# Attention products on two halves of TensorE's columns, in a fused linear-attention and MoE kernel

## What is computed

```
# r, k, v: (4, 8, 768, 48) = batch, head, time, head_dim; w, u: (8, 48)
for t in range(S):
    cur = einsum('bhd,bhe->bhde', u * k_t, v_t)
    y_t = einsum('bhd,bhde->bhe', r_t, state + cur)
    state = w * state + einsum('bhd,bhe->bhde', k_t, v_t)
x = y as 3072 tokens of 384 features
h = max(x @ w1, x @ w2, x @ w3)            # 384 -> 768
x = h @ w_out                              # 768 -> 384
xn = x / sqrt(mean(x * x) + 1e-6) * rms_g
out = (silu(xn @ w_gate) * (xn @ w_val)) @ w_out2     # 384 -> 1536 -> 384
```

## Time and profile before

| | us |
|---|---|
| median of 3 runs | 930.51 |
| lowest and highest run | 929.02, 930.55 |
| span of the profiled execution, first to last instruction | 927.3 |
| TensorE busy in it | 890.9 |
| VectorE, ScalarE, POOL busy | 439.4, 334.9, 156.6 |

### The profile page before, as it was taken

One profiled execution on the slowest core, in us unless ns is written; L12 is line 12 of the kernel. 1 busy time (PEld: TensorE's weight loads), 2 busy tenths in 40 slices (PEclk: granted clock), 3 DMA queues, 4 the chain that ended last, 5 costly groups with the idle time before them and its releaser, 6 DMA issues.

```text
span 927.3 us, 15577 instructions
## 1 busy us (share of the span) xinstructions
PE 890.9 (96%) x5428; PEld 884.9 (95%) x5428; DVE 439.4 (47%) x1053; ACT 334.9 (36%) x790; POOL 156.6 (17%) x197
## 2 busy tenths in 40 slices
PE   3689999999999999999999999999999999999998
PEld 3579999999999999999999999999999999999998
DVE  7976565546555565644532524234342432424321
ACT  2453333434334333333445324333243332433322
POOL 5552223232212223200334100000000000000000
PEclk9779999999999999999999999999999999999999
DMA  7263113122311312103232000000000000000000
GB/s 238 92 213 112 58 56 115 55 62 65 103 54 55 112 54 77 37 6 102 69 80 58 17 10 1 27 1 27 0 0 25 0 25 0 0 25 0 25 1 26
DMA packets 44406, 48.28 MB, mean 52 GB/s; under 512 B 3536, under 2 KB 38224, under 8 KB 44368
## 3 DMA queue, kind: packets, MB, share of 16 engines
q1 hardware_dynamic: 44368, 47.79, 16.5%
HBM read 41.88 MB, written 4.72 MB: 50 GB/s over the span
## 4 chain that ended last, share of the span: by engine, by line
PE 91%; DVE 6%; issue 2%; ACT 0%; DMA 0%; DVEq 0%; ACTq 0%
PE h_b L409 16%; PE h_b L411 16%; PE h_b L410 16%; PE y_b L409 8%; PE y_b L411 8%; PE y_b L410 8%; PE a_b L395 4%; PE s_b L380 4%; PE s_b L409 3%; PE s_b L410 3%; PE s_b L411 3%; PE a_b L399 2%; DVE kd L773 2%; PE a_b L403 1%; DVE xl L807 1%
## 5 line engine op out<-in xcount | busy, mean ns | idle before, releaser
L409 PE MATMUL h_b<-xh,Wh 128*128 128x384 f32 x648 | 225.8, 348 | 4.1 <-DVE xl L807 4.1
L411 PE MATMUL h_b<-xh,Wl 128*128 128x384 f32 x648 | 217.8, 336 | 0.0
L410 PE MATMUL h_b<-xl,Wh 128*128 128x384 f32 x648 | 217.7, 336 | 0.0
L409 PE MATMUL y_b<-hh,Wh 128*128 128x384 f32 x432 | 144.5, 334 | 0.4 <-DVE hl L982 0.3
L411 PE MATMUL y_b<-hh,Wl 128*128 128x384 f32 x432 | 144.6, 335 | 0.0
L410 PE MATMUL y_b<-hl,Wh 128*128 128x384 f32 x432 | 144.3, 334 | 0.0
L409 PEld LDWEIGHTS h_b<-xh,Wh 128*128 128x128 f32 x648 | 122.2, 189 | 5.5 <-issue 4.4
L410 PEld LDWEIGHTS h_b<-xl,Wh 128*128 128x128 f32 x648 | 122.4, 189 | 0.0
L411 PEld LDWEIGHTS h_b<-xh,Wl 128*128 128x128 f32 x648 | 122.1, 188 | 0.0
L709 ACT CAST hh<-hB 128x384 fp32r<-128x384 f32 x96 | 49.4, 514 | 164.7 <-DVE hB L977 163.4
L322 POOL TENSOR_TENSOR rd<-rbuf,PR 112x128 f32<-112x128 f32 x96 | 45.7, 477 | 271.5 <-PE a_b L403 237.8
(11 more groups left out here) (120 smaller groups left out, 1346.6 us busy)
## 6 DMA issues: line engine op xcount, KB each, us to landing
vbuf<-in_v SPq DMA_DIRECT2D x24, 320.0 KB, 4.1
kbuf<-in_kT SPq DMA_DIRECT2D x24, 256.0 KB, 3.5
rbuf<-in_rT SPq DMA_DIRECT2D x24, 256.0 KB, 3.8
rnbuf<-in_r SPq DMA_DIRECT2D x24, 192.0 KB, 2.4
knbuf<-in_k SPq DMA_DIRECT2D x24, 192.0 KB, 2.5
x<-in_wA SPq DMA_DIRECT2D x6, 768.0 KB, 7.4
wst<-in_gv SPq DMA_DIRECT2D x12, 384.0 KB, 3.3
out_t<-xraw SPq DMA_DIRECT2D x7, 576.0 KB, 3.3
```

Source lines behind the costliest of these rows:

```text
L409: nc.tensor.matmul(bank[:, 0:GT], hi, xhi, start=first, stop=False)
L410: nc.tensor.matmul(bank[:, 0:GT], hi, xlo, start=False, stop=False)
L411: return nc.tensor.matmul(bank[:, 0:GT], lo, xhi, start=False, stop=last)
```

## The change

In `attend` each product is made of two matmuls. One writes bank rows 0 to 63 (0 to 47 for the new state), with stationary columns 0 to 63 (0 to 47); the other writes rows 64 to 111, with the 48 columns of the second head. The two products with the values no longer accumulate into each other. The new state's blocks both lie in columns C to C + D of the bank, each on its own rows, and VectorE reads them there.

```diff
@@ attend
                 vv = vbuf[:, j, pair, :]
-                for half in range(2):
-
-                    nc.tensor.matmul(bank[0:R, 0:C], vv[:, half * D:half * D + R], A[:, k % 4, half, :],
-                                     start=(half == 0), stop=(half == 1 and n == 0))
+                for out, columns, half in ((slice(0, HB), slice(0, HB), 0), (slice(HB, R), slice(VP - D, VP), 1)):
+
+                    last = nc.tensor.matmul(bank[out, 0:C], vv[:, columns], A[:, k % 4, half, :],
+                                            start=True, stop=(n == 0))
                 if n > 0:
                     pe.wait_ge(state_ready, updates(i, n - 1, k))
-                    last = nc.tensor.matmul(bank[0:R, 0:C], T[0:R, pair, 0:R], rd[0:R, k % 4, :], start=False, stop=True)
+                    for out in (slice(0, HB), slice(HB, R)):
+                        last = nc.tensor.matmul(bank[out, 0:C], T[0:R, pair, out], rd[0:R, k % 4, :],
+                                                start=False, stop=True)
                 if n < UPD:
                     pe.wait_ge(kn_scaled, UPD * i + n + 1)
-                    heads = bass.AP(vv.tensor, vv.offset, [list(vv.ap[0]), [R, 2], [1, D]])
-                    last = nc.tensor.matmul(bank[0:R, C:C + 2 * D], kn[:, n % 2, pair, 0:R], heads,
-                                            start=True, stop=True)
+                    for out, columns in ((slice(0, D), slice(0, D)), (slice(HB, R), slice(VP - D, VP))):
+                        last = nc.tensor.matmul(bank[out, C:C + D], kn[:, n % 2, pair, out], vv[:, columns],
+                                                start=True, stop=True)
                 last.then_inc(y_ready, 1)
@@ sum_state
-                        new = bank[rows, C:C + D] if at == 0 else bank[rows, C + D:C + 2 * D]
+                        new = bank[rows, C:C + D]
```

## The result

The changed kernel takes 937.22 us (median of 4 runs, 936.91 to 937.50), the kernel before beside it 929.76 us. The ratio is 1.0083, 95% interval 1.0069 to 1.0097: 0.8% slower. Forecast was + 18 us; it became + 7.5 us in the medians and + 8.3 us in the spans. The sign was right, the size not, and the cause is for the most part one that the prediction doesn't name: TensorE waits for its own code.

The account below looks back on a forecast made before the run. TensorE was taken as the bound. Overlap of the halves, - 14 us, and width changes, 32 to 33 us, gave + 18 on a span of 927.3: 945, or 948 us with the 3.2 around it; range 916 to 962.

Parts of the forecast that it names:

- What bounds the kernel: TensorE sets the time, busy 890.9 of 927.3 us; 84 slots lie fully on the path, 12 in part.
- the balance of a slot: In the 84 slots, width changes cost more than overlapping halves save: 32 to 33 us against 14 us.
- the halves overlap: In a slot's products both halves run at once: 0.70 us for 0.88, - 0.18 in a full slot, - 14 us summed.
- The lead of 0.11: At a slot's products, the second half starts no sooner than the first half's second record, costing 0.11 us.
- records start in order: On TensorE, matmul records were taken to start in order, giving the 0.11 us lead of the first half.
- The price of a change of width: Two changes a slot between wide and narrow matmuls: 0.32 us without weight loads, 0.48 with; 27 to 40 us over 84 slots.
- the upper half of 27 to 40: The part of the summed width-change price range that the prediction chose, some 32 to 33 us over 84 slots.
- The prediction's own sign: In a full slot, first L395 to second MoE matmul, 1.05 us before, was to read 1.13 to 1.37.
- The gap between the last score record and L395: Sign of the width-change price ahead of a slot's products: 0.11 us before, should read 0.25 or more.
- full overlap and cheap changes: Rival for the slots: halves overlap and width changes cost little, - 15 us, 915 to 916 us; chance 0.22.

Follow-up runs that it names:

- e7: Changed kernel with all products of the first half, then those of the second, and 61 no-ops to keep the code in place: 943.79 us, ratio 1.0141.
- e4: Kernel before with only the two products with the values on halves, state product and new state one matmul each: 937.85 us, ratio 1.0073.
- e6: Changed kernel with 40 no-ops at the start of TensorE's program: 928.82 us, ratio to the kernel before 0.9989.
- e3: Changed kernel with TensorE's attention loop written out instead of looped: 928.96 us, ratio to the kernel before 0.9986.
- e1: Changed kernel with 112 no-ops at the start of TensorE's program: 928.76 us, ratio to the kernel before 0.9982.
- e9: Kernel before, products unchanged, with 144 no-ops inside TensorE's attention loop and 156 ahead of it: 937.30 us, ratio 1.0071.
- e10: Kernel before, products unchanged, with 144 no-ops inside TensorE's attention loop and none ahead of it: ratio 1.0003.
- e2: Kernel before, loop unchanged, with 234 no-ops ahead of TensorE's attention loop: ratio 0.9996.
- e5: Kernel before, loop unchanged, with 203 no-ops ahead of TensorE's attention loop: ratio 0.9997.

## Why the prediction was wrong

**What bounds the kernel.** Right. No other engine came to set TensorE's pace: the waits from 60 to 430 us are all for issue.

**Two steps failed.** One is the balance of a slot, from which the whole + 18 comes: a price of the changes of width above the overlap's saving, by 0.20 in a full slot. It measured nothing in a full slot. The other is a term that the sum puts at nothing without a reason, the code of a longer loop. They went opposite ways: with the second put right alone, the forecast would have been some + 25 us.

**Overlap or not.** The step "the halves overlap" was right in kind. Its saving, - 0.18 in a full slot, was mis-sized: the saving measured is 0.31 (0.22 on L395; L399's four records for 0.22 against 0.23 for two; L405's 0.085 against 0.17). The lead of 0.11 that I charged rested on "records start in order". They don't: in the changed kernel the two halves' four value records take 0.26 in all, and e7 shows a later half's record ahead of an earlier one.

**The price of a change of width.** Taken as 0.38 a slot, out of bounds of 0.32 and 0.48. e4 gives 0.32, 0.20 of it standing and 0.12 uncovered loads. The stop itself is not 0.16 but 0.10, each way. (The 32 to 33 us that the prediction calls the upper half of 27 to 40 are just below their middle.) The Trainium skill's rule, TensorEngine Tiling (Array Packing), Key Properties, that changing the tiling mode drains TensorE, is borne out in kind by these 0.10 us each way.

Both errors went the same way. A full slot was to lose 0.20 and loses 0; with n = 5, 0.26, and loses 0.12; with n = 0, 0.20, and loses 0. Without the code effect the change is worth - 1.0 to - 1.7 us by the ratios of e6, e3 and e1, and by the table + 0.8 us in the stretch of the slots, against + 18 forecast. The prediction's own sign, the time from the first L395 to the second MoE matmul, reads 0.95 for 1.05; its 1.13 to 1.37 counts both changes of width, though one lies ahead of L395. The gap between the last score record and L395 reads 0.21, 0.10 more than before, where it wanted 0.25. The rival "full overlap and cheap changes" (- 15 us) was nearly as far off on its side: the changes aren't cheap.

**What was missing.** The sum costs 160 more instructions in TensorE's loop at what they take to run, and at nothing for being there. Three waits for code and a fallen clock made 7.3 us, and turned an edit that is near to nothing into a loss. The sign of the forecast came out right for a reason that it doesn't contain. The page had the line of the instruction queue, 22 transfers, and I didn't read it. Its trace has no such transfer from 208 to 440 us. The changed kernel has 18 there, e9 too, and e1 has 1:

```profile
q8 instruction: 18, 0.29, 0.5%
```

So the code of the loop before stayed, and 1577 instructions growing by a tenth should have raised the question whether it still would.

The Trainium skill speaks of this in Runtime: NRT & Kernel Launch, Instruction fetch mechanics: code is fetched ahead in 16 KiB blocks of 256 instructions, TensorE's store holds 128 KiB, and a taken branch to a target outside the current two-page window stalls. The transfers here have that size. A stop at a jump back is what the changed kernel shows; but by a window of two pages the loop before, 1577 instructions long, would stop too, and its trace has no gap and no transfer there. Its 128 KiB would allow 2048 instructions; here 1721 and 1737 lose at some places, and e9 with e10 show that place decides. What the runs don't settle is the edge itself: starts at 1186, 1193 and 1213 lose and one at 1233 doesn't, and my two tries to place it by count failed (e2, e5). That the store's last free block is taken by code fetched ahead is the reading that I hold likely; it was only argued.

## What to carry to other kernels

Adding instructions to a long loop can cost a stop at its jumps back: here 1577 instructions had none, and 1721 or 1737 had one or two at each, or none, by where the loop lay. Compare the count of instruction transfers in the two profiles before explaining a difference by the edit, and move the code by a few no-ops, or write the loop out, to tell the two apart. Halves of the array pay only where enough narrow work stands together: here three products of a slot saved 0.31 us and the two changes of width cost 0.32.

## What was not expected of the hardware

- A change between matmuls of up to 64 and of 112 to 128 columns costs 0.10 us of standing each way, and 0.04 or 0.08 for the weight load that is no longer hidden.
- fp32 matmuls on the two halves run fully at once: four records of 128 moving columns in 0.22 us, where two wide ones take 0.22 or 0.23.
- A matmul on one half starts ahead of earlier ones on the other half, but it came 0.27 us late with six of them before it.
- A wait for code at a jump back, or some us behind it, takes 1.4 to 2.4 us in the changed kernel, and 20 no-ops decide whether it comes: 941.05 us with 20, 928.82 us with 40.
- After the first such stop, of 2.39 us, the granted clock was 0.50 for 3 us; after the second, of 2.26, it stayed at 1.00. In e4 a stop of 1.6 us was followed by 0.57. No run here shows what decides.
